# Where four weight buffers begin modulo 512 bytes, in a chain of attention, mixture of experts and MLP on one core

## The reference

```python
# attention: 4 batches, 8 heads, 576 positions in chunks of 64, head size 64
scores = scale * np.matmul(q_c, k_c.transpose(0, 1, 2, 4, 3))
scores = scores - np.max(scores, axis=-1, keepdims=True)
attn = np.exp(scores)
attn = attn / (np.sum(attn, axis=-1, keepdims=True) + 1e-09)
out = np.matmul(attn, v_c)                 # -> x: 2304 tokens x 512
# mixture of experts: N = 2304, D = 512, E = 8, F = 1024
P = np.exp(logits - logits.max())          # logits = x @ w_gate
for _ in range(8):
    P /= P.sum(1, keepdims=True) + 1e-09
    P /= P.sum(0, keepdims=True) + 1e-09
    P *= N / E
for e in range(E):
    out += P[:, e:e + 1] * (np.maximum(x @ w1[e], 0.0) @ w2[e])
# MLP: 512 -> 2048 -> 512
h = x @ w_in
g = np.where(h > 0.0, h, np.exp(np.minimum(h, 0.0)) - 1.0)
return g @ w_out
```

## Time and profile before

| | us |
|---|---|
| median of 3 runs (lowest, highest) | 2165.11 (2163.65, 2166.01) |
| the profiled execution | 2163.2 |
| its span, first to last instruction | 2161.4 |
| PE busy | 2130.3 (99%) |
| PE weight load busy | 1937.2 (90%) |
| DVE busy | 823.4 (38%) |
| ACT busy | 455.9 (21%) |
| POOL busy | 22.4 (1%) |
| DMA moved | 61.39 MB, 28 GB/s |
| mean granted TensorE clock | 0.994 |

### The profile page before, as it was taken

The page is one execution under the profiler, slowest core; times in us unless marked ns, Lnnn a source line. Parts: engine busy times, 40 slices in busy tenths (PEclk is TensorE's granted clock), DMA queues, the critical chain, the costliest instruction groups (busy, mean ns, idle before and its releaser), DMA issues.

```text
span 2161.4 us, 30934 instructions
## 1 busy us (share of the span) xinstructions
PE 2130.3 (99%) x11248; PEld 1937.2 (90%) x11248; DVE 823.4 (38%) x1439; ACT 455.9 (21%) x882; POOL 22.4 (1%) x29
## 2 busy tenths in 40 slices
PE   6999999999999999999999999999999999999999
PEld 5888899999999999999999999999999989999998
DVE  3444443332333233333333332333233345555544
ACT  3333311111111111111111111111111133223222
POOL 0000003000000000000000000000000000000000
PEclk8999999999999999999999999999999999999999
DMA  5223100000000100000000001000000000000001
GB/s 126 60 59 97 40 20 20 20 20 20 19 19 19 39 19 19 19 19 19 19 19 19 19 19 35 23 19 19 19 19 19 19 20 20 20 20 20 0 30 58
DMA packets 81304, 61.39 MB, mean 28 GB/s; under 512 B 58480, under 2 KB 58480, under 8 KB 81264
## 3 DMA queue, kind: packets, MB, share of 16 engines
q1 hardware_dynamic: 79680, 58.73, 9.0%
q10 hardware_dynamic: 1584, 2.11, 0.3%
HBM read 56.12 MB, written 4.72 MB: 28 GB/s over the span
## 4 chain that ended last, share of the span: by engine, by line
PE 96%; DVE 2%; issue 1%; ACT 1%; DMA 0%; ACTq 0%; SPq 0%; DVEq 0%; POOL 0%; POOLq 0%
PE down_ps L360 29%; PE up_ps L327 22%; PE ab_ps L360 14%; PE ab_ps L327 11%; PE cd_ps L327 11%; PE down_ps L346 2%; PE cd_ps L407 2%; PE up_ps L317 2%; PE cd_ps L385 1%; PE ab_ps L399 1%; PE ab_ps L413 1%; DVE row_max L665 1%; DVE x_row L682 0%; DVE soft L668 0%; PE cd_ps L480 0%
## 5 line engine op out<-in xcount | busy, mean ns | idle before, releaser
L513 ACT ACTIVATE h_hi<-up_ps 128x384 fp32r<-128x384 f32 x204 | 100.4, 492 | 1002.9 <-PE up_ps L327 955.9
L770 DVE SCALAR_TENSOR_TENSOR acc<-down_ps,route,acc 128x512 f32 x168 | 123.9, 751 | 424.0 <-PE down_ps L360 418.4
L651 DVE SCALAR_TENSOR_TENSOR h_lo<-up_ps,h_hi 128x384 fp32r<-128x384 f32 x204 | 113.8, 558 | 301.3 <-ACT h_hi L513 301.3
L360 PE MATMUL down_ps<-w_hi_b,h_lo 128*128 128x512 f32 x480 | 187.7, 391 | 0.0
L360 PE MATMUL down_ps<-w_lo_b,h_hi 128*128 128x512 f32 x480 | 187.4, 390 | 0.0
L360 PE MATMUL down_ps<-w_hi_b,h_hi 128*128 128x512 f32 x480 | 186.9, 389 | 0.0
L360 PE MATMUL down_ps<-w_hi_a,h_lo 128*128 128x512 f32 x432 | 169.0, 391 | 0.0
L360 PE MATMUL down_ps<-w_hi_a,h_hi 128*128 128x512 f32 x432 | 169.0, 391 | 0.0
L360 PE MATMUL down_ps<-w_lo_a,h_hi 128*128 128x512 f32 x432 | 168.7, 391 | 0.0
L327 PE MATMUL up_ps<-x_hi,w_lo_b 128*128 x480 | 161.1, 336 | 0.0
L327 PE MATMUL up_ps<-x_hi,w_hi_b 128*128 x480 | 161.0, 335 | 0.0
(11 more groups left out here) (144 smaller groups left out, 4279.9 us busy)
## 6 DMA issues: line engine op xcount, KB each, us to landing
stage<-in_moe_w SPq DMA_DIRECT2D x30, 1024.0 KB, 5.0
q_raw<-in_q SPq DMA_DIRECT2D x36, 128.0 KB, 2.4
k_raw<-in_k SPq DMA_DIRECT2D x36, 128.0 KB, 2.8
v_raw<-in_v SPq DMA_DIRECT2D x36, 128.0 KB, 2.9
out<-acc SPq DMA_DIRECT2D x18, 256.0 KB, 2.0
stage<-in_moe_w_in SPq DMA_DIRECT2D x4, 1024.0 KB, 5.0
stage<-in_moe_w_out SPq DMA_DIRECT2D x4, 1024.0 KB, 5.1
stage<-in_moe_w ACTq DMA_DIRECT2D x2, 1024.0 KB, 8.8
```

The source lines that it names most:

```text
L360: mm = nc.tensor.matmul(y_ps[j], h, w, start=f == 0 and n == 0, stop=f == FT - 1 and n == 2)
L513: nc.scalar.activation(h_hi[:, f, :], bank, ACT.Relu).then_inc(h_hi_done, 1)
L651: nc.vector.scalar_tensor_tensor(h_lo[:, f, :], bank, 0.0, h_hi[:, f, :].bitcast(F32), ALU.max, ALU.subtract).then_inc(h_lo_done, 1)
L770: nc.vector.scalar_tensor_tensor(acc_tile(t), y_ps[j], route_flat[:, bass.ds(EXPERTS * t + expert, 1)], acc_tile(t), ALU.mult, ALU.add).th ...
```

## The change

The two buffers in the arena and the two behind it are placed anew. `place[0]` is moved on by 32 bytes ahead of w_hi_b and by 352 bytes between w_hi_b and w_lo_b (together 384, and with the two buffers 33,152 bytes, which the arena holds). A filler of 256 bytes stands between w_hi_a and w_lo_a, and another behind w_lo_a. All tensors behind that lie 512 bytes further on. `place[0]` is set back to the arena's start for the tiles of attention as before.

```diff
+        place[0] += 32
         w_hi = [sb("w_hi_a", [P, 2, KT, FW], F32R), at_arena("w_hi_b", [P, 2, KT, FW], F32R)]
-        w_lo = [sb("w_lo_a", [P, 2, KT, FW], F32R), at_arena("w_lo_b", [P, 2, KT, FW], F32R)]
+        sb("shift_lo_a", [P, P // 2])
+        w_lo_a = sb("w_lo_a", [P, 2, KT, FW], F32R)
+        sb("shift_rest", [P, P // 2])
+        place[0] += 352
+        w_lo = [w_lo_a, at_arena("w_lo_b", [P, 2, KT, FW], F32R)]
         place[0] = arena_at
```

## The result

The changed kernel takes 2173.32 us (5 runs, 2172.95 to 2174.17), the kernel before in the same comparison 2164.45 us (5 runs, 2163.45 to 2166.01): a ratio of 1.0041 with a 95% interval of 1.0026 to 1.0056. It is 8.9 us slower. Against the medians of the kernel before in the comparisons further down (2163.96, 2163.46 and 2163.60 us, 13 runs each) it would be 9.4 to 9.9 us. The forecast was 2165.1 us and no change, with a range up to 2172.0; it was wrong, and on the side of rival B.

What follows compares the result with a forecast made beforehand. PE was taken to bound the kernel, its time being matmul count times step. All parts summed to 0 us, leaving the 2161.4 us span; 1.8 and 1.9 us on top gave 2165.1 us, range 2160 to 2172.

Steps and rivals of the forecast that it cites:

- rival B: In `down`, streaming w_hi_b 32 bytes past a multiple of 64 costs 13.3 ns on 1,440 matmuls: 19 us, 2184 us; chance 0.11.
- What bounds the kernel, and the question: PE, busy 99% of the span; only whether a matmul's step depends on its operands' places modulo 512 matters.
- ACT, DVE and DMA at nothing: Writing weight pieces and DMAs: 0 us, since PE's work hides the pieces; at most 110 us without that cover.
- A weight load at another place than the stream, taken at 0: On PE, a load placed differently modulo 512 from the stream beside it: 0, bounds -13.3 to +13.3 ns per matmul.
- rival A: In `up` and `down`, 13.3 ns per matmul is a same-place collision, vanishing for 6,720 matmuls: 89 us, 2076 us; chance 0.08.
- The moving operand, taken at 0 as "the weakest step": In `down`, weight buffers streamed from another place: 0, bounds 0 and +13.3 ns per matmul.
- The constant of 13.3 ns: In every `up` and `down` matmul, the step's time beyond one column per cycle of 2.4 GHz: about 13.3 ns.
- A rival in which a new distance costs: In `up` and `down`, 13.3 ns more on every pair with new places: 89 us, 2254 us; chance 0.02.
- The two independent read ports: On PE, separate ports for stream and weight load, from the skill page: no placement could gain anything.

## Why the prediction was wrong, point by point

**What bounds the kernel, and the question:** right. The same 11,248 matmuls run, PE stays busy for 99% of the span, and in the loops the change acts through the step alone.

**ACT, DVE and DMA at nothing:** right. In the changed kernel the pieces take 624 to 627 ns on ACT and 692 ns on DVE (medians), the latter as before, and DVE's wait for `down_ps` is even 422.0 us. Weight loads stay at 0.188 us: a price on a pair does not show in the load's own row.

**A weight load at another place than the stream, taken at 0:** this step failed. It rested on one step of 0.17 us beside the load of e_wide. First, the timeline shows starts to 0.01 us, while 0.2% of the time is 4.3 us / 10,080 = 0.43 ns per matmul. Two rows that agree to 10 ns can exclude the loss of the whole 13.3 ns, and so rival A, but not a mean price of 0.9 ns in `up` and 3.4 ns in `down`, which is what was paid. The prediction itself named 0.5 ns as what would make it wrong, and its evidence could not see that. Second, a finer reading of the same rows would not have helped: the starts in ns give 173 for both steps. The steps vary, and with w at 96, the distance of e_wide, a block of `up` either runs evenly at 173 to 174 ns or alternates between 175 and 179 ns, 8.33 or 8.48 us in all. One step is no sample, and 96 was none of the new places. Third, the steps with 512 columns are the last of their stretch: in ns they are 231 before e_wide and 232 before acc, after steady steps of 226 to 227, so the end of a stretch adds 4 to 5 ns at either place and hides what the place does. What the runs showed in its place: 45 ns per block of `up` on b, 0.9 ns for each of its 48 matmuls.

**The moving operand, taken at 0 as "the weakest step":** this failed too. It is 121 ns per block of `down` on b, 3.4 ns for each of its 36 matmuls and the larger part of the loss, within the bounds of 0 and 13.3 ns. The rows on v_raw and gate_w could not tell, as was said. Both terms are one: in `up` the weight buffer is the load, in `down` the stream, and what has a price is the distance between the two.

**Rival A** did not come true. The constant of 13.3 ns is in the mean step of every kernel, at whatever distance; no block of any had a mean step under 173.2 or 226.6 ns.

**Rival B** had the sign, and `down` on b as the larger part, but a wrong mechanism: with every operand 32 bytes further on nothing is lost. Its 19 us stood against 8.9. That the loss goes by the pair was seen in the arithmetic of rival A (the 60 x 84 matmuls on b with a new distance), only with the sign turned. A rival in which a new distance costs was given 0.02, and only at the full 13.3 ns.

**The two independent read ports.** The Trainium skill, page "SBUF — State Buffer", section "Who interferes with whom", gives PE one read port for the moving operand and an independent one for the weight load. By it stream and load should not feel each other, and this counted against rival A. The runs differ: with x alone moved by 32 bytes the mean step of `up` is 3.3 ns longer over the 173.3 of even steps, at the same loads and streams. The measurement decides.

**What stays open.** Why a distance costs what it does stays open. The runs fix that it is a matter between the stream and the load beside it, that a distance of 256 bytes costs nothing in the two cases tried (w_lo, x), that the sign counts, that prices do not add, and that equal places can run at two rates. Whether all distances repeat at 256 is not settled: w at 224 and at 480 agree in `down` (8.389 us) and in the first pass of `up` (8.484), but not in the later passes (8.321 against 8.484). A collision in SBUF fits these, but no row shows one, and distances below 32 bytes were not tried, nor h moved by itself.

## What to carry to other kernels

Where one engine runs back to back and the time is a count times a step, work out first how small a step's change would decide, and rest nothing on rows that are coarser than that: average over a block. Where matmuls of fp32r follow each other with a new weight load for each, the distance between the streamed and the loaded buffer is worth a scan in steps of 32 bytes, since buffers that happen to share one place lost 1.2% here when one of each two was moved by 32 or 384 bytes (2188.9 and 2190.6 us); a filler ahead of the buffer that is streamed alone (x here) is the cheapest thing to try, and its gain of 0.3% came from the steps after a change of loop.

## What the runs showed of the hardware that I had not expected

- The mean step of a matmul depends on the place of the weight load beside it relative to its own stream. For 384 columns the steady steps have a mean of 173.3 ns at a distance of 0, 176.7 with the stream 32 bytes on, and 173.3 with the load 32 bytes on. The durations of the loads stay at 188 ns.
- A shift of x by 256 bytes gives the kernel before back: blocks of 16.547 us on b.
- The slow steps after a change between `up` and `down`, 0.07 us per block, are for the most part no price of the change of shape. With x at 480, 7 ns of them are left (16.487 us per block against 16.480 of even steps).
- The same matmuls on the same places can run at two rates in one execution, 8.48 and 8.32 us for 48, and hold either for a pass (w_hi_a and w_lo_a at 224).
